# Sparse attention with two feed-forward layers: where ACT's copies stand among the exponentials, and the first two units of each second layer in turn

## What is computed

```python
scores = scale * np.matmul(q, k.transpose(0, 1, 3, 2))
kth = np.partition(scores, -top_k, axis=-1)[..., -top_k:-top_k + 1]   # top_k = 32
scores = np.where(scores >= kth, scores, -1000000000.0)
attn = np.exp(scores - np.max(scores, axis=-1, keepdims=True))
attn = attn / (np.sum(attn, axis=-1, keepdims=True) + 1e-09)
x = np.matmul(attn, v)                # then (tokens, 512)
h = x @ w_in                          # first layer
y = np.maximum(0.01 * h, h) @ w_out
h = y @ w_in                          # second layer, its own weights
g = np.where(h >= 1, h, np.where(h <= -1, 0.0, (h + 1) ** 2 / 4))
out = g @ w_out
```

## Time and profile before

| | us |
|---|---|
| median of 3 runs | 1182.33 |
| lowest, highest | 1179.64, 1183.82 |
| the profiled execution | 1177.87 |
| span of its instructions | 1176.1 |
| PE busy | 1097.9 |
| DVE busy | 900.4 |
| ACT busy | 769.1 |
| POOL busy | 462.9 |

### The profile page before, as it was taken

One profiled execution on the slowest core, in us unless ns is written; L12 is line 12 of the kernel. 1 busy time (PEld: TensorE's weight loads), 2 busy tenths in 40 slices (PEclk: granted clock), 3 DMA queues, 4 the chain that ended last, 5 costly groups with the idle time before them and its releaser, 6 DMA issues.

```text
span 1176.1 us, 21510 instructions
## 1 busy us (share of the span) xinstructions
PE 1097.9 (93%) x7568; PEld 1006.8 (86%) x7568; DVE 900.4 (77%) x2209; ACT 769.1 (65%) x1683; POOL 462.9 (39%) x493
## 2 busy tenths in 40 slices
PE   5458998899999999999999989999999999999998
PEld 3236888699988899899998879988998999999998
DVE  7999999989899998999979989988994006300334
ACT  6777889777678877777768758677875224322232
POOL 5545458552254422543325434224532233222222
PEclk9668999999999999999999999999999999999999
DMA  6868989787656688788766657565466677887774
GB/s 212 323 245 304 410 308 327 250 333 272 228 195 249 233 308 285 264 288 294 243 237 240 221 204 256 195 218 177 172 211 212 208 256 245 268 275 254 250 243 141
DMA packets 90682, 295.53 MB, mean 251 GB/s; under 512 B 10064, under 2 KB 13776, under 8 KB 90576
## 3 DMA queue, kind: packets, MB, share of 16 engines
q1 hardware_dynamic: 86544, 289.45, 70.6%
q10 hardware_dynamic: 4032, 4.72, 1.1%
HBM read 255.85 MB, written 38.27 MB: 250 GB/s over the span
## 4 chain that ended last, share of the span: by engine, by line
PE 67%; DVE 23%; ACT 5%; POOL 2%; issue 2%; DMA 1%; POOLq 0%; SPq 0%; ACTq 0%; DVEq 0%
PE ps_f L906 18%; PE ps_f L914 18%; PE ps_f L907 17%; DVE top L1178 10%; DVE work L1181 9%; PE ps_av L865 6%; PE ps_s L826 2%; DVE part_r L1211 2%; PE ps_t L842 2%; PE ps_t L826 1%; PE ps_t L848 1%; POOL gate L719 1%; DMA raw<-wd 1%; ACT probs L1023 1%; ACT probs L1015 1%
## 5 line engine op out<-in xcount | busy, mean ns | idle before, releaser
L1178 DVE MAX8 top<-work 128x8 f32<-128x576 f32 x432 | 310.9, 746 | 0.1
L906 PE MATMUL ps_f<-xy,w_ring 128*128 128x384 f32 (+2 forms) x896 | 290.8, 325 | 4.8 <-ACT xy L1097 3.6
L914 PE MATMUL ps_f<-xy,w_ring 128*128 128x384 f32 (+2 forms) x896 | 282.8, 316 | 2.9 <-POOL xy L729 2.8
L906 PE MATMUL ps_f<-gate,w_ring 128*128 128x384 f32 (+2 forms) x896 | 285.1, 318 | 0.0
L914 PE MATMUL ps_f<-gate,w_ring 128*128 128x384 f32 (+2 forms) x896 | 280.5, 313 | 3.8 <-POOL gate L719 3.7
L907 PE MATMUL ps_f<-xy,w_ring 128*128 128x384 f32 (+2 forms) x896 | 281.3, 314 | 0.0
L907 PE MATMUL ps_f<-gate,w_ring 128*128 128x384 f32 (+2 forms) x896 | 279.7, 312 | 0.0
L1181 DVE MATCH_REPLACE8 work<-top,work 128x576 f32<-128x576 f32 x288 | 214.1, 743 | 0.0
L719 POOL TENSOR_TENSOR gate<-part_r,gate 128x384 fp32r<-128x384 f32 (+2 forms) x112 | 100.6, 899 | 242.9 <-ACT gate L1082 242.7
L906 PEld LDWEIGHTS ps_f<-xy,w_ring 128*128 128x128 f32 x896 | 170.6, 190 | 20.1 <-issue 10.6
L914 PEld LDWEIGHTS ps_f<-xy,w_ring 128*128 128x128 f32 x896 | 170.8, 191 | 5.5 <-POOL xy L729 4.9
(11 more groups left out here) (84 smaller groups left out, 1848.1 us busy)
## 6 DMA issues: line engine op xcount, KB each, us to landing
w_ring<-w_split SPq DMA_DIRECT2D x408, 512.0 KB, 4.3
w_split<-w_ring SPq DMA_DIRECT2D x40, 512.0 KB, 6.9
raw<-wd SPq DMA_DIRECT2D x64, 256.0 KB, 5.0
w_split<-xy SPq DMA_DIRECT2D x24, 512.0 KB, 4.4
v_sb<-vd SPq DMA_DIRECT2D x32, 320.0 KB, 4.5
kq<-kqd SPq DMA_DIRECT2D x16, 480.0 KB, 5.7
kq<-kqd SPq DMA_DIRECT2D x15, 416.0 KB, 3.4
out_t<-y_acc ACTq DMA_DIRECT2D x12, 192.0 KB, 4.4
```

What stands on the lines that cost most here:

```text
L906: pe.matmul(out, w[:, 0, m], high, start=first, stop=False)
L914: mm = pe.matmul(out, w[:, 0, m], low, start=False, stop=end)
L1178: dve.max(top[:, t % T_SLOTS, 8 * r:8 * r + 8], source(t, r)).then_inc(dve_step, 1)
```

## The change

ACT's order in the steps from 21 on: `copy_scores` (where it stood behind) now stands ahead of `exponential(t)`, and in the steps with a `soon` tile `copy_values` and `copy_transposed` stand ahead of `exponential(soon)`. On PE the first two hidden units of each second layer (`TWINS`, seven pairs) are worked in turn: sources 0 to 2 of the first, sources 0 to 2 of the second into its own bank, then source 3 of the first; the second one's source 3 stays where the second unit stood.

```diff
--- before.py
+++ after.py
@@ -363,6 +363,15 @@
 EARLY_UNITS = UNITS[:BANKS]
 
 
+def opens_run(u):
+    return u.i == 0 and not (u.hidden and u.block)
+
+
+TWINS = {u.n: UNITS[u.n + 1] for u in HIDDEN if u.layer and opens_run(u)}
+SECONDS = {second.n for second in TWINS.values()}
+assert all(UNITS[n].segment == second.segment and second.i == 1 for n, second in TWINS.items())
+
+
 def next_needs(u):
     return UNITS[u.n + 1].needs if u.n + 1 < len(UNITS) else len(UNITS)
 
@@ -893,7 +902,7 @@
                     else:
                         source = GATE_OF[u.segment, b]
                         high, low, out = gate_of(source, 0), gate_of(source, 1), bank(u)
-                    opens = u.i == 0 and not (u.hidden and u.block)
+                    opens = opens_run(u)
                     gp = u.chunk.last_gp - CK + 1 + b
                     if opens and u.hidden and not u.layer:
                         pe.wait_ge(x_high_done, gp + 1)
@@ -923,7 +932,16 @@
                 if u.n < len(EARLY_UNITS):
                     products(u, [CK - 1])
                     return
+                if u.n in SECONDS:
+                    products(u, [u.sources - 1])
+                    return
                 open_bank(u)
+                if u.n in TWINS:
+                    products(u, range(u.sources - 1))
+                    open_bank(TWINS[u.n])
+                    products(TWINS[u.n], range(u.sources - 1))
+                    products(u, [u.sources - 1])
+                    return
                 products(u, range(u.sources))
 
             pe.wait_ge(ident_ready, 1)
@@ -1140,23 +1158,23 @@
                     keep(t)
                 for u in first:
                     event(u)
-                if t is not None:
-                    exponential(t)
                 if not scores_first(s):
                     for it in SCORED_AT[s]:
                         copy_scores(it)
+                if t is not None:
+                    exponential(t)
                 if s + 1 in OUT_AT:
                     normalise(OUT_AT[s + 1])
                 if soon is not None:
                     keep(soon)
                 for u in second:
                     event(u)
-                if soon is not None:
-                    exponential(soon)
                 if s in VALUES_AT and not hurried(VALUES_AT[s]):
                     copy_values(VALUES_AT[s])
                 if done:
                     copy_transposed(done)
+                if soon is not None:
+                    exponential(soon)
                 for u in third:
                     event(u)
                 if s in VALUES_AT and hurried(VALUES_AT[s]):
```

## The result

| | median us | lowest to highest | runs |
|---|---|---|---|
| before | 1182.33 | 1179.64 to 1183.82 | 5 |
| changed | 1172.34 | 1169.04 to 1174.02 | 5 |
| changed, a second time, beside 1179.39 us for before (11 runs) | 1170.88 | 1169.57 to 1174.07 | 6 |

The ratio to before is 0.9934 (95% interval 0.9908 to 0.9959), and in the second measurement 0.9929 (0.9911 to 0.9948): 8 us faster. The medians of the first two rows lie further apart, by 10.0 us (a quotient of 0.9916); the recorded ratio is used here, and the second measurement, with more runs, bears it out (8.5 us between its medians). The forecast was 1174.6 us, 0.9935. The total came out as forecast, its terms did not; most of what follows is on that.

What follows compares the result with a forecast made beforehand. PE was taken as the bound from 210 us, except in DVE's stretches at second layers. Stalls of 6.0 us plus 1.7 us of clock made 7.7 us off 1177.87, scaled to 1174.6 us; range 1169.5 to 1181.0 us.

Steps and rivals of the forecast that it cites:

- chunk 0: Second layer's opening in chunk 0: stalls of really 2.2 us exceed the cover of nine matmuls; gain 1.03 us.
- step 37 swapped: ACT's copy of transposes ahead of the exponential in step 37 comes sooner for PE's scores at 207.70 us: gain 0.76 us.
- chunk 1: Second layer's opening in chunk 1: really 1.3 us of stalls covered, but DVE is the bound to 386 us: gain 0.
- chunk 4: Second layer's opening in chunk 4: really 2.1 us of stalls, gain 1.55 us on the path.
- rival (c): DVE takes PE's gains back before 636 us: only 1.1 to 2.7 us kept, 1179.6 to 1181.2 us; chance 0.22.
- Part 2: ACT's copies ahead of the exponential, in 26 steps and steps 36 to 38: gain 0.76 us, all at step 37.
- step 38's lateness: Late exponential makes DVE stand 1.2 us in step 38; idle time covers it, cost 0; 2.5 us with step 42 if uncovered.
- The clock: Drops behind the stalls at 479 and 807 us cost about 1.7 us each; one counted as gone, 1.7 us.
- rival (a): Both clock drops, at 479 and 807 us, go with the stalls: 9.4 us faster, 1172.9 us; chance 0.20.
- Rival (b): The stalls go but the clock drops stay or move: 6.0 us faster, 1176.3 us; chance 0.16.
- Rival (d): ACT idles before late scores with the exponential undone, five steps, 4.4 us: 5.8 us slower in all, 1188 us; chance 0.05.
- Rival (e): PE's going between two banks brings a clock drop at all seven openings: 5.9 us slower, 1188 us; chance 0.02.

Runs made afterwards that it cites:

- copies alone: ACT's copies of scores, values and transposes moved ahead of the exponentials, PE's order unchanged, against the kernel before: 1178.98 us, ratio 0.9993.
- chunk 1 alone: First two hidden units worked in turn in chunk 1's second layer only, ACT's order as before, against the kernel before: 1179.47 us, before 1179.39.
- part 1 alone: First two hidden units of each second layer worked in turn, ACT's order as before, against the kernel before: 1172.87 us, ratio 0.9945.
- step 38 ahead: The changed kernel with the exponential of step 38 back ahead of the copies of values and transposes: 1172.74 us, ratio 0.9940 to the kernel before.
- scores alone: Only the copies of the scores moved ahead of the exponential, in 26 steps, against the kernel before: 1180.26 us, ratio 1.0007.
- seven ahead: On step 38 ahead: block 1's first two output units in turn too, seven of eight sources ahead: 1168.39 us (0.9910 to before); again, 1169.52 us.
- five ahead: On step 38 ahead: block 1's first two output units in turn, chunks 3, 4 and 6 only, five sources ahead: 1164.90 us, 0.9871 to before.
- outputs of both blocks: As seven ahead, with the first two output units of each second layer's first block in turn too: 1169.26 us, ratio 0.9913 to before.

## Why the prediction was right, step by step

The time, 1172.34 us, lies in the range and 2.3 us under the forecast. The sum behind the forecast was 6.0 us of stalls and 1.7 of clock. The trace and the runs give about 3.5 us of stalls, and the clock the rest. Two errors cancelled, so that the total came out within 2.3 us is luck; the direction and the first mechanism, filling PE's waits, are not.

**The stalls,** predicted and then read from the table (changed kernel; a drop of the clock taken out by the column in which it alone is gone, copies alone for chunk 2, chunk 1 alone for chunk 4):

| | predicted | measured |
|---|---|---|
| chunk 0 | 1.03 | 1.09, of which 0.38 is back by 199 us: 0.71 |
| step 37 swapped | 0.76 | 0.76 |
| behind step 41: late exponential, step 38 | 0 | -0.85 |
| copies of the scores | 0 | -0.3 |
| chunk 1 | 0 | 1.30 - 1.28 = 0 |
| chunk 2 | 1.03 | 2.56 - 1.47 = 1.09 |
| chunk 3 | 0.5 | 0.5 |
| chunk 4 | 1.55 | 3.0 - 1.5 = 1.5, of which 1.34 is back by 876 us: 0.2 |
| chunks 5 and 6 | 1.1 | 0.68 + 0.68 = 1.4 |
| sum | 6.0 | 3.5 |

The changed kernel's second trace, which has no drop, checks the sum another way: behind the first row it wins 8.68 us, and what before lost by its four drops is 0.53 + 1.47 + 1.66 + 1.44 = 5.1 us, each from a column in which it is gone and nothing else changes at that place; 3.6 us remain.

The size of each filled stall was right: idle time plus a hidden part of 0.15 to 0.2 us at each (chunks 5 and 6: 0.3), up to the cover of nine matmuls. Three steps failed.

*Chunk 4 was taken for PE's.* "Elsewhere from 210 us on the chain is PE's" held in the profile before and not in the one after. The stretch behind chunk 4's opening, before and then after:

```profile
815.00:868.00 53.00, 53.00 (x357) 48.02 (x356) 51.16 (x122) 44.00 (x97) 23.55 (x24) 1.00 0.54 185
```
```profile
811.00:866.00 55.00, 54.03 (x359) 48.75 (x359) 54.44 (x133) 45.29 (x98) 24.21 (x24) 1.00 0.55 183
```

DVE had 1.84 of 53 us to spare. With PE 3 us earlier (stall and clock together) the spare time was used up: DVE is busy for 54.44 of 55 us and PE waits. The kernels with twins in chunk 4 all give back 1.0 to 1.4 us there; chunk 1 alone, where only the drop is gone (1.45 us), gives back nothing. That was rival (c), true for this one chunk.

The chain of waits says it too. From 806.25 to 834.5 us it lies on DVE's lines in the changed kernel, and it ends in a wait of PE, by which 0.88 of the 1.34 us go (the other 0.46 go at 817.42 us, where PE waits for ACT's `p_rem`):

```profile
833.47 1.04 DVE part_r L1229
834.51 0.07 issue
834.58 1.01 POOL part_o L734
835.59 0.98 POOL gate L728
836.57 0.04 issue
836.61 0.44 PE ps_f L923
```

*Part 2 was worth nothing, not 0.76 us, and step 38's lateness was put at nothing,* with a price of 2.5 us "if that cover were gone". The cover was read over too long a stretch. DVE's 8 us of idle time in 215 to 318 us all lie behind 230 us; where the late row sum falls, DVE has none (before):

```profile
214.00:230.00 16.00, 14.13 (x123) 13.66 (x124) 15.95 (x42) 13.34 (x30) 5.01 (x5) 1.00 0.92 334
```

So DVE is later by its wait of 1.02 us, and the chain of waits of the changed kernel goes from that row sum at 215.65 us along DVE's lines to 229.95 us, then over POOL to chunk 1's x at 235.68 us, for which PE waits 1.54 us. By that 0.85 us of what PE had won is lost.

The 0.76 us of step 37 were no gain by themselves either. With step 38's exponential ahead, 0.56 of them go at 212 us, where PE waits for ACT again: a swap in ACT's order brings one copy sooner, and the next copy behind both comes when it did. Part 2 as a whole is nothing (0.9993).

The forecast for the wait at 207 us failed as well, 1.61 us where "some 0.6" stands: chunk 0's 1.03 us did not fit into it. In the kernel with part 1 alone that wait is 2.36 us as before, and what chunk 0 won is still there behind it (+1.38 ahead of the wait, +1.39 behind): ACT's copy had come sooner with PE. DVE's wait in step 38 (1.02 us) came as forecast; in step 42 it was 0.60 us where over 2 was forecast; in the kernel with step 38 ahead, where DVE is not held up before, it was 2.01.

*The clock was put too low.* Forecast and rival (a) differed in whether one or both drops go. Both went. Here are the twelve traces:

| drop of the granted clock | kernels without twins there | with twins there |
|---|---|---|
| at 480 us (chunk 2) | 3 of 4 | 0 of 8 |
| at 806 us (chunk 4) | 3 of 4 | 0 of 8 |
| at 690 us (chunk 3's outputs) | 7 of 8 | 1 of 4 |

Without twins in the first two rows are before, copies alone, scores alone and chunk 1 alone; with twins among the outputs in the third are seven ahead (both runs), five ahead, and the outputs of both blocks, whose trace has the one drop. One drop is worth 1.45 to 1.7 us in these columns, but that at 231 us only 0.53 (before beside scores alone; in part 1 alone and chunk 1 alone too): PE without it waits 1.16 us for x right behind. Over many runs: the profile of each run lists its mean granted clock, and time x (1 - clock) is what PE lost by it. On the chip of the second measurement that is 29.0 us of 1180.0 (mean of 11 runs of before) and 22.8 us of 1171.4 (6 runs of the changed kernel): of 8.6 us some 6.1 go with the clock, 2.5 with the rest. For part 1 alone it is 4.5 of 6.5. Not all of the clock's loss lies on the path, above all in the first 100 us, so 6 us is more than the clock's share; the 3.5 us of stalls leave 8 - 3.5 = 4.5 us for it. Rival (a)'s mechanism is the one that happened; the forecast was saved by the stalls being worth less.

Rival (b) is refuted by the drops. Rival (d): ACT did stand idle with the exponential undone, and it cost 0.3 us (the wait at 453 us), not 4.4; ratio 1.0007. The signs set for (c) and (d): DVE's last `top` starts at 886.8 us, before at 891.0, so attention does end sooner. Rival (e): the kernel that goes to and fro between banks most, outputs of both blocks, has one drop behind the start in its trace and a mean clock of 0.979 (6 runs) against 0.9755 for before. By the rule of the Trainium skill cited there ("TensorE: Matmul & The Clock Gate", section "A second HAM failure mode: psum-queue depth-cycling") it should have been the lowest; no run here agrees with it.

**What stays open.** Why chunk 0 gives back 0.38 us around 190 us (PE waits 1.24 us for ACT's `part_o` at 192.19 us, 1.03 in the kernel with the copies alone) was not tried. Nor was the chain behind PE's wait for `p_rem` at 817 us followed to its start, nor whether the clock's drops are caused by the stalls or by what both have in common; filling a stall and losing its drop were never separated.

## What to carry to other kernels

A stall of PE on the last operand of an accumulation can be filled with the next unit's products into another bank, at no cost but the later end of the first unit: fill it only where the profile shows the wait, and put the moved work ahead of the source that is late, not ahead of the last one. (With 7 sources ahead 0.991, with 5 ahead and only at three chunks 0.987; 2.75 of the 3.5 us between the two traces come from the sources, 0.8 from the chunks.) Before a gain is booked, look for the engine with the second highest busy share in the stretch behind it: its spare time there bounds what is kept (1.84 of 53 us, and 1.66 of 3.0 us were kept). And a delay is not free because its engine is idle on average: read the spare time in the few us behind the late result (0.05 of 16 us here, not 8 of 103). A gain from swapping two instructions of one engine wants the same care: look for the next wait for that engine.

## What the runs showed of the hardware

Where the granted clock drops differs between executions of one kernel: of the two traces of the changed kernel one has two drops (at 689 and 884 us) and the other none behind 103 us. Behind the start, drops were seen in twelve traces at 209, 231, 480, 690, 806 and 884 us (a few us to and fro), once at 172 us, and nowhere else. Each came at or behind waits of PE of together 1.4 to 2.4 us; but the same waits passed without a drop in other executions. Each lasts 3.4 us, once 6.8 (copies alone, at 806 us). One costs 1.45 to 1.7 us, and 0.53 us at 231 us, where PE would have waited. Here is one at 690 us, in part 1 alone, and behind it the same stretch in the second trace of the changed kernel; columns as in the earlier trace rows:

```profile
690.00:694.00 4.00, 3.74 (x14) 2.12 (x16) 3.96 (x14) 3.01 (x7) 1.03 (x2) 0.57 0.29 104
```
```profile
690.00:694.00 4.00, 4.00 (x35) 2.96 (x32) 4.00 (x12) 2.68 (x6) 0.87 (x1) 1.00 0.84 319
```

The other surprise is how much of a change of 0.7% was the clock's: the stalls gave 3.5 us, and 4.5 us or more came from PE being longer at the upper level.
